# Written-out attention steps with two score buffers, and VectorE clamps every tile's forget logits in place of GpSimd

## The reference, cut to what matters

```python
def _attn_ref(q, k, v, f_logit):            # (4, 8, 768, 48) each
    f = 1.0 / (1.0 + np.exp(-f_logit))
    state = zeros((B, H, D, D))
    for t in range(S):
        state = f[:, :, t, :, None] * state + einsum('bhd,bhe->bhde', k[:, :, t], v[:, :, t])
        y[:, :, t] = einsum('bhd,bhde->bhe', q[:, :, t], state)

x = y.transpose(0, 2, 1, 3).reshape(3072, 384)
logits = x @ w_gate + modality_bias[modality_id]        # 8 experts, top 1
out[mask_e] = gate[mask_e] * (relu(x[mask_e] @ w1[e]) @ w2[e])
# then, on every token: RMS norm, silu(xn @ w_gate2) * (xn @ w_val) @ w_out
```

## Time and profile before

| | |
|---|---|
| time, median of 3 runs | 869.16 us (864.9 to 869.27) |
| profiled execution | 866.84 us |
| its span | 865.1 us, 15457 instructions |
| PE busy | 833.0 us, 96% |
| DVE busy | 471.8 us, 55% |
| ACT busy | 389.6 us, 45% |
| POOL busy | 165.6 us, 19% |
| chain that ended last | PE 78%, issue 2%, DVE 1% |

### The profile page before, as it was taken

How to read it: one execution, slowest core, us unless ns; L and a number is a source line. 1 busy time by engine, 2 the same in 40 slices (tenths; PEclk the granted TensorE clock), 3 DMA queues, 4 the chain that set the end, 5 groups by cost and what they waited for, 6 DMA issues and landing times.

```text
span 865.1 us, 15457 instructions
## 1 busy us (share of the span) xinstructions
PE 833.0 (96%) x5332; PEld 762.5 (88%) x5332; DVE 471.8 (55%) x773; ACT 389.6 (45%) x750; POOL 165.6 (19%) x165
## 2 busy tenths in 40 slices
PE   6999999779999999989999999999999999999997
PEld 6798988779999999989888888888888898888887
DVE  7989898687766666653444333334333333433332
ACT  5988786375666555653423411331241133123112
POOL 5444352318554000000000200100020010001001
PEclk9999999889999999999999999999999999999999
DMA  9877666497988797750200200100020000000000
GB/s 182 188 148 169 150 146 210 153 387 239 301 258 260 245 344 255 255 147 20 74 1 1 74 0 1 66 8 0 0 73 0 0 28 8 0 0 36 0 0 36
DMA packets 44082, 96.49 MB, mean 112 GB/s; under 512 B 9168, under 2 KB 25040, under 8 KB 43920
## 3 DMA queue, kind: packets, MB, share of 16 engines
q1 hardware_dynamic: 39952, 85.81, 33.6%
q0 software_dynamic: 3840, 9.47, 3.1%
q10 hardware_dynamic: 256, 0.79, 0.4%
HBM read 76.75 MB, written 19.29 MB: 111 GB/s over the span
## 4 chain that ended last, share of the span: by engine, by line
PE 78%; issue 2%; DVE 1%; POOL 0%; ACT 0%; DVEq 0%; ACTq 0%
PE h_ps L1779 16%; PE h_ps L1781 15%; PE h_ps L1780 15%; PE ym_ps L1779 7%; PE ym_ps L1781 7%; PE ym_ps L1780 7%; PE xTm_ps L1780 3%; PE xTm_ps L1779 3%; PE xTm_ps L1781 3%; PE xT_ps L1796 1%; PE xTm_ps L1787 1%; POOL out L1443 0%; DVE h_lo L1691 0%; DVE w_lo L1664 0%; ACT w_hi L1461 0%
## 5 line engine op out<-in xcount | busy, mean ns | idle before, releaser
L1754 DVE TENSOR_TENSOR gs<-h_ps,sig 128x512 f32<-128x512 f32 x72 | 49.8, 691 | 175.5 <-ACT sig L1555 175.5
L1555 ACT ACTIVATE sig<-h_ps 128x512 f32<-128x512 f32 x72 | 43.1, 598 | 158.9 <-PE h_ps L1781 158.9
L1566 ACT CAST h_hi<-hid 128x512 fp32r<-128x512 f32 x72 | 44.6, 620 | 150.2 <-DVE hid L1757 150.2
L1779 PE MATMUL h_ps<-x_hi,w_hi 128*128 128x256 f32 x312 | 89.7, 287 | 7.7 <-DVEq L1682 5.1
L1781 PE MATMUL h_ps<-x_lo,w_hi 128*128 128x256 f32 x312 | 89.3, 286 | 0.0
L1780 PE MATMUL h_ps<-x_hi,w_lo 128*128 128x256 f32 x312 | 89.1, 285 | 0.0
L1779 PE MATMUL h_ps<-w_hi,wg_hi 128*128 128x512 f32 x216 | 85.5, 396 | 0.0
L1781 PE MATMUL h_ps<-w_lo,wg_hi 128*128 128x512 f32 x216 | 84.6, 392 | 0.0
L1781 PE MATMUL h_ps<-w_lo,wv_hi 128*128 128x512 f32 x216 | 84.2, 390 | 0.0
L1780 PE MATMUL h_ps<-w_hi,wv_lo 128*128 128x512 f32 x216 | 84.0, 389 | 0.0
L1779 PE MATMUL h_ps<-w_hi,wv_hi 128*128 128x512 f32 x216 | 84.0, 389 | 0.0
(11 more groups left out here) (222 smaller groups left out, 1890.0 us busy)
## 6 DMA issues: line engine op xcount, KB each, us to landing
w_raw<-in_w SPq DMA_DIRECT2D x52, 384.0 KB, 5.0
w_in<-in_w SPq DMA_DIRECT2D x52, 384.0 KB, 5.1
qkf_in<-in_qkf SPq DMA_DIRECT2D x43, 288.0 KB, 5.0
y_sorted<-x_group SPq DMA_DIRECT2D x13, 384.0 KB, 3.4
v_in<-in_v SPq DMA_DIRECT2D x24, 192.0 KB, 4.3
x_regions<-zero_row SPq DMA_DIRECT2D x12, 384.0 KB, 2.9
x_group<-x_regions SPq DMA_DIRECT2D x12, 384.0 KB, 3.9
g_in<-in_wg SPq DMA_DIRECT2D x3, 768.0 KB, 8.1
```

The source lines that it names most:

```text
L1555: nc.scalar.activation(sig[:], g_ps, ACT.Sigmoid).then_inc(sig_done, 1)
L1566: nc.scalar.copy(h2_hi[:, fb % HELD], hid[:]).then_inc(h2_hi_done, 1)
L1754: nc.vector.tensor_tensor(gs[:], g_ps, sig[:], ALU.mult).then_inc(gs_done, 1)
L1779: nc.tensor.matmul(out, hi, rhs_hi, start=first, stop=False)
```

## The change

- `steps` writes every step out for all engines; loops, branches and the argument `more` go.
- `sc_ps` has two buffers. The score product waits for the mask of two tiles before; the read waits for the mask of its own tile.
- `x_ps` has one bank in place of two, and the routing counts lie in its free columns. The x product waits for the logits of the tile just before. The last tile's x goes to the bank of `yT_ps`, and tile 23's read to that of `ks_ps`.
- VectorE clamps tile n + 2 behind the logits reduction of step n; GpSimd no longer does.
- The counting moves from the end of a chunk's last step to the first step of the next, ahead of x.
- Transposes, growth, state and copies use 112 rows or columns (ROWS) in place of 128. Transposes, `ks` copies, growth, sums and states of the last four tiles are left out, since nothing reads them.
- One pick, in the first step of the last chunk, in place of two. SP waits for it and loads the weights ahead of the last two v loads.
- At the end the early rows are turned ahead of tile 23's read, and one w1 split moves behind the block into `experts`.

```diff
...
-        sc_ps = ps("sc_ps", [P, 2, PR, P])
+        sc_ps = ps("sc_ps", [P, 2, 2, PR, P])
...
-        x_ps = ps("x_ps", [P, 2, 512])
-        rt_ps = ps("rt_ps", [P, 3, E])
-        flag_ps = rt_ps[:, 2, 0:1]
+        x_ps = ps("x_ps", [P, 512])
+
+        def x_pairs(n):
+            bank = yT_ps[:].rearrange("p j t -> p (j t)") if n == NT - 1 else x_ps
+            return bank[:, 0:PR * XG].rearrange("p (j r) -> p j r", j=PR)
+
+        rt_ps = x_ps[:, PR * XG:PR * XG + 2 * E].rearrange("p (i e) -> p i e", i=2)
+        flag_ps = ds_ps[:, DM:DM + 1]
...
-            for i in range(2 * B):
-                step(i // B, i % B, i // B, nullcontext)
-            with eng.Fori(1, CH // 2) as i:
-                for half in range(2):
-                    for b in range(B):
-                        step(i * 2 + half, b, half, (lambda: eng.If(i < CH // 2 - 1)) if half else nullcontext)
+            for c in range(CH):
+                for b in range(B):
+                    step(c, b, c % 2)
...
+            sp.wait_ge(ahead_sems.picked, 1)
+            e = first.expert_of(sp)
+            first.load_weights(sp, e, w1, w2, ahead_sems)
             for b in range(2):
                 load_v(*tile(CH, b, 2))
-
-            sp.wait_ge(ahead_sems.picked, PICKS)
-            e = first.expert_of(sp)
-            first.load_weights(sp, e, w1, w2, ahead_sems)
...
-            def clamp(c, b):
-
-                pool.wait_ge(qkf_landed[b], (c + 1) * 32)
-                pool.sem_inc(ordered, 1)
-                f = qkf_in[:, b, 2]
-                nc.gpsimd.tensor_scalar(f, f, LEAST_LOGIT, None, ALU.max).then_inc(clamped, 1)
...
-                if t := tile(c, b, 1):
+                if (t := tile(c, b, 1)) and t[2] < GROWN:
                     _, s, n = t
                     act.wait_ge(k_turned, n + 1)
                     wait_past(act, ds_done, n - 3)
-                    nc.scalar.copy(ks[:, s], ks_ps[:]).then_inc(ks_done, 1)
+                    nc.scalar.copy(ks[:, s, :, 0:ROWS], ks_ps[:, :, 0:ROWS]).then_inc(ks_done, 1)
...
+                if t := tile(c, b, -2):
+                    dve.wait_ge(qkf_landed[t[1]], (t[0] + 1) * 32)
+                    f = qkf_in[:, t[1], 2]
+                    nc.vector.tensor_scalar(f, f, LEAST_LOGIT, None, ALU.max).then_inc(clamped, 1)
...
-                    if half and not at(c, CH):
-
-                        first.pick(nc, dve, rt, ahead_sems, (c - 3) * (Ahead.PICKED // 2))
+                    if c == CH - 1:
+                        first.pick(nc, dve, rt, ahead_sems, 0)
...
+            def read(c, b, t, acc):
+                cc, s, n = t
+                pe.wait_ge(masked, n + 1)
...
+                if n < GROWN and n > 0:
+                    growth(s, n)
+
+                wait_past(pe, state_done, n - 3)
+                if not at(cc, 0):
+                    for j in range(PR):
+                        nc.tensor.matmul(acc[0:ROWS, j], state[0:ROWS, s, j, 0:ROWS], qT[0:ROWS, s, j], start=(j == 0), stop=False,
+                                         skip_group_check=True)
...
-                    wait_past(pe, ks_done, n)
-                    for j in range(PR):
-                        mm = nc.tensor.transpose(ks_ps[:, j], kT[:, s, j], ident[:])
-                    mm.then_inc(k_turned, 1)
+                    if n < GROWN:
+                        wait_past(pe, ks_done, n)
+                        for j in range(PR):
+                            mm = nc.tensor.transpose(ks_ps[:, j, 0:ROWS], kT[0:ROWS, s, j], ident[0:ROWS, 0:ROWS])
+                        mm.then_inc(k_turned, 1)
...
-                    wait_past(pe, masked, n)
+                    wait_past(pe, masked, n - 1)
...
+                if at(c, CH) and b == 1:
+                    pe.wait_ge(ks_done, GROWN)
+                    read(c, b, tile(c, b, 2), ks_ps)
...
                 if t := tile(c, b, 3):
...
                     pe.wait_ge(yT_kept, n + 1)
-                    wait_past(pe, x_kept, n - 1)
+                    if n < NT - 1:
+                        wait_past(pe, x_kept, n)
+                    if c > 1 and b == 0:
+                        pe.wait_ge(rt_made, RT_MADE)
+                        pe.wait_ge(marks, (c - 2) * Routing.PLACED + Routing.CHOSEN)
+                        rt.count(nc, rt_ps[:, 0], rt_ps[:, 1]).then_inc(counted, 1)
...
+                if at(c, CH) and b == 0:
+                    first.turn(nc, pe, xT_ps, ident, ahead_sems)
...
-            dve.sem_inc(w1_split, GR)
+            dve.sem_inc(w1_split, GR - 1)
             dve.sem_inc(x_split, 1)
             rt.choose(nc, dve, CH - 1, marks, 0)
+            lo_w1(0, GR - 1)
             lo_w2(0, 0)
```

More of the change, by code:

```diff
@@ L489, in _, with step @@
                                     pattern=[[1, P]], channel_multiplier=-1).then_inc(rt_made, 1)
-            def clamp(c, b):
-                pool.wait_ge(qkf_landed[b], (c + 1) * 32)
-                pool.sem_inc(ordered, 1)
-                f = qkf_in[:, b, 2]
-                nc.gpsimd.tensor_scalar(f, f, LEAST_LOGIT, None, ALU.max).then_inc(clamped, 1)
[L498 to L501, removed]
+            def step(c, b, half):
                 if not (at(c, 0) or at(c, 1)):
@@ L510, in step @@
                     rt.scatter(nc, half, b, x_regions).then_inc(ended if at(c, CH) else scattered[b], 16)
-            pool.sem_inc(clamped, FIRST_TWO)
-            steps(pool, step)
+            steps(step)
             for b in range(B):
@@ L530, in neg_logs, with step @@
                 nc.scalar.activation(neg_log[:, b % 2, :, 1:P + 1], exp_f[:], ACT.Ln, bias=1.0).then_inc(log_done, 1)
-            def step(c, b, half, more):
+            def step(c, b, half):
                 if t := tile(c, b, 0):
@@ L542, in step @@
                 if (t := tile(c, b, -1)) and not (at(c, 0) and b == 0):
-                    with ahead(b, 1, more):
-                        neg_logs(*t)
-                if t := tile(c, b, 1):
+                    neg_logs(*t)
+                if (t := tile(c, b, 1)) and t[2] < GROWN:
                     _, s, n = t
@@ L567, in step, with kept @@
                     nc.scalar.copy(rt.x[:, slot, s, :].rearrange("p (j r) -> p j r", j=PR),
[L568 to L575, removed]
-                if at(c, CH) and b == 0:
[L577 to L581, removed]
+                                   x_pairs(n)[:, :, 0:2 * D]).then_inc(x_copied, 1)
+                if at(c, CH) and b == 0:
+                    for g in range(2):
+                        first.hi_w1(nc, act, g, ahead_sems)
+                if (t := tile(c, b, 2)) and not (at(c, CH) and b == 1):
+                    kept(t, yT_ps)
+                if at(c, CH) and b == 0:
+                    first.hi_w1(nc, act, 2, ahead_sems)
+            def kept(t, acc):
+                _, s, n = t
+                act.wait_ge(y_done, n + 1)
+                wait_past(act, x_done, n - 1)
+                nc.scalar.copy(yT[0:ROWS, s % 2], acc[0:ROWS]).then_inc(yT_kept, 1)
             nc.scalar.preload_act_table_set("natural_log_exp_and_others")
@@ L589, in _ @@
                 neg_logs(0, b, b)
-            steps(act, step)
+            steps(step)
         @block.vector
@@ L619, in step @@
                 if (t := tile(c, b, -1)) and not (at(c, 0) and b == 0):
-                    with ahead(b, 1, more):
-                        sums(*t)
+                    sums(*t)
                 if t := tile(c, b, 1):
@@ L704, in _ @@
             dve.wait_ge(consts, CONSTS)
-            steps(dve, step)
+            dve.sem_inc(clamped, FIRST_TWO)
+            steps(step)
         @block.tensor
@@ L777, in step @@
-                if b == B - 1 and not (at(c, 0) or at(c, CH)):
-                    pe.wait_ge(rt_made, RT_MADE)
-                    pe.wait_ge(marks, (c - 1) * Routing.PLACED + Routing.CHOSEN)
-                    rt.count(nc, rt_ps[:, 0], rt_ps[:, 1]).then_inc(counted, 1)
-                if at(c, CH) and b == 1:
-                    pe.wait_ge(small_ready, 1)
-                    nc.tensor.matmul(flag_ps, rt.ones_r[:], small[:], start=True, stop=True).then_inc(flag_sum, 1)
+                if (t := tile(c, b, 2)) and not (at(c, CH) and b == 1):
+                    read(c, b, t, yT_ps)
@@ L785, in step @@
+                if at(c, CH) and b == 0:
                     first.turn(nc, pe, xT_ps, ident, ahead_sems)
-            steps(pe, step)
+            steps(step)
 def general_attention(nc, qkf, v, w_gate, ident, rt, first, w1, w2, x_rows, flag, x_regions):
@@ L1005, in _ @@
                 first.pick(nc, dve, rt, again, 0)
-                for g in range(GR):
+                for g in range(GR - 1):
                     first.lo_w1(nc, dve, g, again)
```

81 lines of the change are left out of this document (36 added, 45 removed).

## The result

The kernel after the change takes 860.11 us (median of 15 runs, 857.94 to 863.03), the kernel before, on the same chip, 868.67 us (15 runs, 864.0 to 870.87): ratio 0.9906, interval 0.9893 to 0.9919.

The account below looks back on a forecast made before the run. In attention TensorE bounds plain steps and VectorE routing steps, taking turns with waits. Steps 4.2 plus tail 2.5 gave 6.7 us: 860.1 against the profiled 866.84, 862.5 against the median; range 857 to 868.5.

Parts of the forecast that it names:

- The main term: steps of attention: Attention, tile 4 to tile 23: fewer waits between engines gain 4.2 us, bounds 0.5 and 7.4.
- 0.25 us of waiting in nine steps, 2.3 us: VectorE in attention: after plain steps the scan waits for the logarithm, as the clamp holds the exponential; 2.3 us added.
- 0.9 for hand-overs: VectorE, tile 4 to tile 23: 0.9 us added for hand-overs that no profile row shows.
- TensorE stays just under VectorE's 5.5: Attention steps: TensorE needs 5.36 us a plain step, VectorE's mean step with clamp and routing is 5.5.
- The x bank's wait: TensorE in attention: x waits for the previous tile's logits; a 10.3 us loop per two steps, capping only plain runs.
- The picks: VectorE in attention: removing the earlier of two expert picks takes away 2.1 us of work.
- Stretches against clamps: VectorE, tile 4 to tile 23: 3.9 us of operations stretched by GpSimd's clamps go, 6.1 us of own clamps come.
- Up to tile 4, loops: Early attention: four clamps (1.4 us) against equal waits, no gain; written-out loops: nothing, at most 0.5 us gained.
- The tail: Attention's end after tile 23's kT: last scatters come earlier through dropped work; gain 2.5 us, bounds -0.5 to +3.5.
- The clamp never met a scatter: Rival for attention: 16 scatters each hold up a VectorE clamp, 14 us added; 870 to 875 us, slower, chance 0.10.
- Rival 2: Attention and tail: waits only move, most of the 6.9 us stays; 865 to 869 us, within 0.5%, chance 0.28.
- Rival 3: Attention through hand-over: VectorE hardly waits, TensorE keeps its clock; 857 us or a little below, chance 0.12.

Follow-up runs that it names:

- the two clamp runs: Clamps moved to VectorE in the kernel before: 868.85 us, ratio 0.999; clamps moved back to GpSimd in the kernel after: 862.33 us, ratio 0.9931.
- the repeat: The kernel after, unchanged, timed and profiled once more: 862.07 us, ratio 0.9925 to the kernel before.
- the loop and the 128-row experiments: Kernel before with its sixteen middle steps written out: 870.03 us, ratio 1.0014; kernel after with 128 rows and columns again: 862.55 us, ratio 0.9933.

## Why the prediction was right, and where its terms were not

**The main term: steps of attention.** 4.2 us foretold, 5.25 and 4.45 measured in the two profiles. Part of that is the clock's: the four steps from tile 12 to tile 16, with the dip, take 26.08 in the profile before and 24.16 at full clock with the loops written out. By this estimate 1.9 us are the dip that the prediction left in its bounds at up to 1.7, and 3.3 are the change's, somewhat less than foretold. That the waits, not the work, could be gained held: VectorE's waits from tile 4 to T were 6.4 us before (6.9 by the prediction's sum; 2.6 of them are the two waits behind the dip) and are 1.7 after; its plain step with clamp is 4.78 for 4.75, TensorE's 5.38 for 5.36, the clamp 0.43 in a slot of 0.34 to 0.35.

**The mis-sized term: "0.25 us of waiting in nine steps, 2.3 us", and "0.9 for hand-overs".** VectorE waited in just nine steps: six times 0.16 for the logarithm, three times 0.26 for `rise`, 1.74 in all. Counted with the overlap of 0.08 that a wait takes away, each logarithm wait costs the foretold 0.24, each `rise` wait 0.34, together 2.5 where 3.2 stood; the 0.9 had no row behind it, and none shows it. But these are not the bound that I took them for. "TensorE stays just under VectorE's 5.5" was wrong by a little: in four steps VectorE's own work is 4 x 4.78 + 1.59 for choosing + 1.10 for placing = 21.8, TensorE's 21.96 and its one wait of 0.41. The run without clamps shows it: with 1.36 less on VectorE, 0.37 came back. The x bank's wait, which the prediction let pass because its loop is 5.15, comes after a choice, where a mean loop says nothing.

**The picks.** 2.1 us foretold, 1.5 measured. The row of 0.73 beside a scatter was in that price; in the kernel after the same instruction took 0.22.

**Stretches against clamps.** 3.9 less and 6.1 more were foretold on VectorE; both occurred, and they do not reach the time by more than some tenths, as the two clamp runs show. The prediction kept them in one sum with the gains, where they stood as part of VectorE's work.

**Up to tile 4, loops.** Nothing foretold, -0.26 us and, by the run of its own, nothing.

**The tail.** 2.5 us foretold, 2.8 and 1.7 measured, with each mark within 1.1 us of its place; the second has x of tile 21 1.0 us later behind its stretch of low clock (132 to 140). Its cause was right in part. The x product of tile 21 came forward by 2.6 us (T + 5.66 to T + 3.06), and the prediction put that down to the work left out. Of it the last tiles' growth and state give 0.75 (and 0.76 more in step 22), but 1.07 is the second score buffer's, and the rest was not undone by itself. The moved SP order, priced at nothing or a loss, keeps TensorE's chain from ending the tail later, by some 0.9.

**Behind attention.** Nothing foretold; 1.1 us less in the first profile, none in the second (705.13 against 705.12). The first work of the experts ran at a granted clock of 0.60 from 152 to 156 and 0.97 from 156 to 160 there, and at 0.72 and 0.50 in the repeat, so this goes with the clock and not with the change.

**The rivals.** The clamp never met a scatter: a clamp starts 0.22 us behind its reduction and is over 0.65 behind its start; the scatter that waits for the logits of 129.82 started at 130.81. Rival 2, that the wait only moves, is true of TensorE: from tile 4 to T it waited 5.0 us for masks before and 5.6 for logits after (0.41 or 0.54 ahead of each counting, the rest in the first two steps and behind the pick). What paid is that its own step is shorter and VectorE's waits are fewer. Rival 3's time, 857, is what reordering growth comes near to (858.5).

**The granted clock.** The forecast was 6.7 us for a measured 8.6, and it left the clock out of the sum. At a mean granted clock of 0.988 seven runs of the kernel before (on the two chips of the loop and the 128-row experiments) average 866.6 us, and six of the 15 of the kernel after 860.4: some 6 us. The other 2 to 2.5 go with a higher mean clock, a median of 0.988 in the kernel after against 0.984 to 0.986 in the runs of the kernel before beside the experiments. The repeat of the kernel after had 0.986, so whether the change itself raises the clock stays open. The range held either way; that the median lies 2.4 us below the forecast is the clock's doing rather than the steps'.

**By part.** What the undoing of one part costs: second score buffer 1.7 to 2.4; 112 columns 1.0; pick 1.5; last tiles 1.5; SP order some 0.9. Together 6.6 to 7.3 us, against some 6 at equal clock and 8.6 between the medians. Each is small beside the spread of the runs; they rest on the steps of the profiles, one profile each, and the timed ratios (0.9933 to 0.9954 for the runs with one of these parts undone) agree in sign with 0.9906 and 0.9925, though all of their intervals overlap with the latter's.

## What to carry to other kernels

Where two engines take turns, sum each one's own work over a whole period of the pattern, not a plain step and not a mean: the engine with the larger sum is the floor (here TensorE, 21.96 against 21.8 in four steps), and the time above the floor is that engine's waits (0.41). Before a difference of some tenths of a microsecond between two profiles is read as an effect, the same kernel should be profiled twice, and the granted clock compared in the stretch in question. After a step that makes the other engine late, ask which of its results is needed first; give that one a buffer, and produce the next early in its step: moving one addition of 0.7 us behind the reduction was worth as much as taking 1.4 us of work away. A transfer moved ahead of one that waits for a buffer can give more than the risk it brings.

## Of the hardware, not expected

The granted clock falls to 1.2 GHz (a share of 0.50) for some 3 to 7 us at places that differ between runs of one kernel. In the kernel after, no stretch from 8 to 150 us was below full clock in the first profile; in the second the clock was at 0.50 from 16 to 20 and 0.66 from 132 to 136. The 15 runs follow their mean granted clock: 857.94 at 0.996, 863.03 at 0.984. In each of the twelve profiles with a dip between tile 4 and T, TensorE had waited 0.9 to 2.0 us, and the clock fell within 2 us behind that wait. But the same wait need not bring a dip: x waited 1.97 us until 130.16 in the first profile of the kernel after and 1.96 us until 131.67 in the second, and only in the second did the clock fall, at 133. What decides it stays open.

A GpSimd clamp cost VectorE 0.4 us at most once for each meeting, whether GpSimd's own operation lasted 1.5 or 2.5 us.
